# A two-MLP kernel after clustered attention: the reciprocal's correction on VectorE alone, weight splits moved between engines

## What is computed

```python
def _moe_ref(x, w_in, w_out, a, b):          # 1536 tokens, d_model 512, d_ff 2048
    h = x @ w_in
    P = a[0] + a[1]*h + a[2]*h*h + a[3]*h*h*h
    Q = 1.0 + abs(b[0])*abs(h) + abs(b[1])*h*h
    g = P / (Q + 1e-06)
    return g @ w_out

def _moe2_ref(x, w_gate, w_val, w_out):      # d_ff 1536
    g = x @ w_gate
    return (g / (1 + exp(-g)) * (x @ w_val)) @ w_out
```

## Time and profile before

| | us |
|---|---|
| median of three runs | 919.03 |
| the three runs | 916.78, 919.03, 922.4 |
| profiled execution, span of its instructions | 917.6 |
| TensorE matmul busy | 838.3 (91%) |
| VectorE busy | 575.2 (63%) |
| ScalarE busy | 475.2 (52%) |
| GpSimd busy | 417.9 (46%) |

### The profile page before, as it was taken

How to read it: one execution, slowest core, us unless ns; L and a number is a source line. 1 busy time by engine, 2 the same in 40 slices (tenths; PEclk the granted TensorE clock), 3 DMA queues, 4 the chain that set the end, 5 groups by cost and what they waited for, 6 DMA issues and landing times.

```text
span 917.6 us, 12016 instructions
## 1 busy us (share of the span) xinstructions
PE 838.3 (91%) x4210; PEld 710.1 (77%) x4210; DVE 575.2 (63%) x885; ACT 475.2 (52%) x898; POOL 417.9 (46%) x404
## 2 busy tenths in 40 slices
PE   5799889898999898888999899789999999999998
PEld 4698778888988676666888687667888888888886
DVE  2799888899999678877777778874322222122222
ACT  3588678777888576667666776753100100010001
POOL 3477787877758876656566666660000000000000
PEclk9999999999999999999999999999999999999999
DMA  3544323232332150000000023223000100010001
GB/s 95 150 112 106 90 69 91 67 100 68 93 82 61 61 169 1 1 0 1 1 1 0 1 70 94 79 69 103 1 1 1 46 0 1 1 46 1 0 1 46
DMA packets 44011, 45.38 MB, mean 49 GB/s; under 512 B 5040, under 2 KB 34736, under 8 KB 43952
## 3 DMA queue, kind: packets, MB, share of 16 engines
q1 hardware_dynamic: 43952, 44.62, 17.3%
HBM read 27.30 MB, written 3.15 MB: 33 GB/s over the span
## 4 chain that ended last, share of the span: by engine, by line
PE 47%; DVE 22%; POOL 12%; ACT 11%; issue 6%; POOLq 0%; DMA 0%; DVEq 0%; SPq 0%; ACTq 0%
PE ps L765 7%; PE ps L766 7%; PE ps L767 7%; POOL mag L373 6%; DVE den L619 4%; DVE neg_max L699 4%; PE ps L879 4%; PE ps L839 4%; PE ps L840 4%; PE ps L841 4%; DVE probT_lo L719 3%; POOL den L368 2%; ACT inv L480 2%; ACT inv L482 2%; DVE num L623 2%
## 5 line engine op out<-in xcount | busy, mean ns | idle before, releaser
L765 PE MATMUL ps<-x_hi,w_hi 128*128 128x512 f32 x480 | 187.1, 390 | 0.0
L766 PE MATMUL ps<-x_lo,w_hi 128*128 128x512 f32 x480 | 186.8, 389 | 0.0
L767 PE MATMUL ps<-x_hi,w_lo 128*128 128x512 f32 x480 | 186.7, 389 | 0.0
L666 DVE TENSOR_TENSOR act<-act,ps 128x512 f32<-128x512 f32 x36 | 24.8, 688 | 208.1 <-PE ps L767 206.1
L496 ACT ACTIVATE act<-ps 128x512 f32<-128x512 f32 x36 | 21.6, 599 | 243.0 <-PE ps L767 243.0
L373 POOL TENSOR_TENSOR mag<-mag,inv 128x512 f32<-128x512 f32 x48 | 81.4, 1695 | 79.6 <-ACT inv L482 79.6
L765 PE MATMUL ps<-g_hi,w_hi 128*128 128x512 f32 x192 | 79.0, 412 | 33.7 <-DVE g_lo L647 25.9
L395 POOL TENSOR_SCALAR prob<-prob,row_inv 128x768 f32<-128x768 f32 x96 | 85.7, 908 | 50.2 <-DVE row_inv L711 50.0
L719 DVE TENSOR_TENSOR probT_lo<-ps,probT_hi 128x384 fp32r<-128x384 f32 x192 | 97.4, 548 | 12.4 <-ACT probT_hi L528 12.0
L879 PE MATMUL ps<-ident,prob 128*128 128x128 f32 x576 | 82.9, 280 | 24.2 <-DVE probT_lo L719 22.4
L765 PEld LDWEIGHTS ps<-x_hi,w_hi 128*128 128x128 f32 x480 | 90.4, 188 | 18.8
(11 more groups left out here) (99 smaller groups left out, 1680.3 us busy)
## 6 DMA issues: line engine op xcount, KB each, us to landing
w_raw<-in_moe_w_out SPq DMA_DIRECT2D x28, 256.0 KB, 4.4
k_hihi<-qkT SPq DMA_DIRECT2D x32, 192.0 KB, 3.0
qk_low<-qkT SPq DMA_DIRECT2D x32, 192.0 KB, 3.7
w_raw<-in_moe_w_in SPq DMA_DIRECT2D x16, 256.0 KB, 3.9
qk_raw<-in_q SPq DMA_DIRECT2D x16, 192.0 KB, 2.7
qk_raw<-in_k SPq DMA_DIRECT2D x16, 192.0 KB, 2.6
v_raw<-in_v SPq DMA_DIRECT2D x16, 192.0 KB, 3.2
w_raw<-in_moe_w_gate SPq DMA_DIRECT2D x12, 256.0 KB, 3.0
```

The source lines that it names most:

```text
L765: mm(dst, hi, m_hi, start=start, stop=False)
L766: mm(dst, hi, m_lo, start=False, stop=False)
L767: return mm(dst, lo, m_hi, start=False, stop=stop)
```

## The change

The two corrections of the reciprocal are arranged anew. GpSimd keeps only den·mag. VectorE makes the product (den + 1 + 1e-6)·inv in one operation (`s_resid`), then inv = (that - 2)·inv, then g as before. ScalarE computes the magnitude and the linear part before num, and num gets a third buffer, with new waits for the shorter-lived buffers. The splits of ten first-MLP and twelve second-MLP weights leave ScalarE: the high part is a VectorE copy at the end of its step, and the low part is a subtraction by GpSimd behind its den·mag of that step. The core of the diff:

```diff
-    num = [place(f"num{i}", [P, TB]) for i in range(2)]
+    num = [place(f"num{i}", [P, TB]) for i in range(3)]
...
 # GpSimd, mlp1(n)
-                pool.wait_ge(s_lin, n + 1)
-                did(g.tensor_tensor(den[i][:, :], den[i][:, :], mag[i][:, :], ALU.mult), s_quad)
-                pool.wait_ge(s_quad, n + 1)
-                did(g.tensor_scalar(mag[i][:, :], den[i][:, :], DEN0, 1.0, ALU.add, ALU.mult), s_den1)
-                pool.wait_ge(s_den1, n + 1)
-                pool.wait_ge(s_inv0, n + 1)
-                did(g.tensor_tensor(mag[i][:, :], mag[i][:, :], inv[i][:, :], ALU.mult), s_newt)
+                if n < N1:
+                    pool.wait_ge(s_lin, n + 1)
+                    did(g.tensor_tensor(den[i][:, :], den[i][:, :], mag[i][:, :], ALU.mult), s_quad)
+                for u, when in w1_split_at.items():
+                    if when == n:
+                        pool.wait_ge(s_w1hi, u - POOL_UNITS + 1)
+                        did(g.tensor_tensor(w1_lo[u][:, :], w1_raw[u][:, :], w1_hi[u][:, :].bitcast(F32),
+                                            ALU.subtract), s_w1lo)
+                for j, when in w2_split_at.items():
+                    if when == n:
+                        pool.wait_ge(s_w2hi, j + 1)
+                        did(g.tensor_tensor(w2_lo[j][:, :], w2_raw[j][:, :], w2_hi[j][:, :].bitcast(F32),
+                                            ALU.subtract), s_w2lo)
...
 # ScalarE, mlps(n)
                     if n >= 2:
-                        sc.wait_ge(s_glo, n - 1)
+                        sc.wait_ge(s_quad, n - 1)
                     hid = ps[:, HID + n % 4, :]
-                    s.activation(num[i][:, :], hid, ACT.Identity, scale=a_neg[:, 3:4],
-                                 bias=a_neg[:, 2:3]).then_inc(s_num, 1)
                     s.activation(mag[i][:, :], hid, ACT.Abs).then_inc(s_mag, 1)
                     sc.wait_ge(s_mag, n + 1)
+                    if n >= 2:
+                        sc.wait_ge(s_inv1, n - 1)
                     s.activation(den[i][:, :], mag[i][:, :], ACT.Identity, scale=b_abs[:, 1:2],
                                  bias=b_abs[:, 0:1]).then_inc(s_lin, 1)
+                    if n >= 3:
+                        sc.wait_ge(s_glo, n - 2)
+                    s.activation(num[n % 3][:, :], hid, ACT.Identity, scale=a_neg[:, 3:4],
+                                 bias=a_neg[:, 2:3]).then_inc(s_num, 1)
...
-                for u, when in w1_split_at.items():
-                    if when == n:
-                        sc.wait_ge(s_w1_in[u], 32)
-                        s.activation(w1_hi[u][:, :], w1_raw[u][:, :], ACT.Copy).then_inc(s_w1hi, 1)
...
                     sc.wait_ge(s_quad, n + 1)
+                    if n >= 2:
+                        sc.wait_ge(s_g, n - 1)
                     s.activation(inv[i][:, :], den[i][:, :], ACT.Ln, bias=den0).then_inc(s_log, 1)
...
 # VectorE, mlps(n)
-                    ve.wait_ge(s_newt, n)
-                    v_.scalar_tensor_tensor(out=den[i1][:, :], in0=mag[i1][:, :], scalar=-2.0,
+                    i1, k1 = (n - 1) % 2, (n - 1) % 3
+
+                    ve.wait_ge(s_inv0, n)
+                    v_.scalar_tensor_tensor(out=den[i1][:, :], in0=den[i1][:, :], scalar=DEN0,
+                                            in1=inv[i1][:, :], op0=ALU.add, op1=ALU.mult
+                                            ).then_inc(s_resid, 1)
+                    ve.wait_ge(s_resid, n)
+                    v_.scalar_tensor_tensor(out=inv[i1][:, :], in0=den[i1][:, :], scalar=-2.0,
                                             in1=inv[i1][:, :], op0=ALU.add, op1=ALU.mult
                                             ).then_inc(s_inv1, 1)
...
                 for u, when in w1_split_at.items():
                     if when == n:
-                        ve.wait_ge(s_w1hi, u - POOL_UNITS + 1)
-                        v_.tensor_tensor(w1_lo[u][:, :], w1_raw[u][:, :], w1_hi[u][:, :].bitcast(F32),
-                                         ALU.subtract).then_inc(s_w1lo, 1)
+                        ve.wait_ge(s_w1_in[u], 32)
+                        v_.tensor_copy(w1_hi[u][:, :], w1_raw[u][:, :]).then_inc(s_w1hi, 1)
```

More of the change, by code:

```diff
@@ L177, in build_program @@
         "s_w1p_hi", "s_w1p", "s_w1hi", "s_w1lo", "s_w2hi", "s_w2lo"))
-    s_hid, s_num, s_mag, s_lin, s_num1, s_num2, s_quad, s_den1, s_log, s_inv0, s_newt = (
+    s_hid, s_num, s_mag, s_lin, s_num1, s_num2, s_quad, s_log, s_inv0, s_resid = (
         sem(x) for x in ("s_hid", "s_num", "s_mag", "s_lin", "s_num1", "s_num2", "s_quad",
-                         "s_den1", "s_log", "s_inv0", "s_newt"))
+                         "s_log", "s_inv0", "s_resid"))
     s_inv1, s_g, s_ghi, s_glo, s_y, s_yhi, s_ylo = (sem(x) for x in (
@@ L428, in _ @@
                     mlp1(TAIL[step])
-            for n in range(len(TAIL), N1):
+            for n in range(len(TAIL), N1 + N2 + 2):
                 mlp1(n)
@@ L474, in mlps @@
                         sc.wait_ge(s_y, n - 3)
-                    s.activation(g_hi[(n - 1) % 3][:, :], num[(n - 1) % 2][:, :], ACT.Copy
+                    s.activation(g_hi[(n - 1) % 3][:, :], num[(n - 1) % 3][:, :], ACT.Copy
                                  ).then_inc(s_ghi, 1)
@@ L615, in mlps @@
                 if 1 <= n <= N1:
-                    i1 = (n - 1) % 2
-                    ve.wait_ge(s_newt, n)
-                    v_.scalar_tensor_tensor(out=den[i1][:, :], in0=mag[i1][:, :], scalar=-2.0,
+                    i1, k1 = (n - 1) % 2, (n - 1) % 3
[5 more added lines that the diff above has]
+                    v_.scalar_tensor_tensor(out=inv[i1][:, :], in0=den[i1][:, :], scalar=-2.0,
                                             in1=inv[i1][:, :], op0=ALU.add, op1=ALU.mult
@@ L622, in mlps @@
                     ve.wait_ge(s_inv1, n)
-                    v_.scalar_tensor_tensor(out=num[i1][:, :], in0=num[i1][:, :], scalar=a_neg[:, 0:1],
-                                            in1=den[i1][:, :], op0=ALU.add, op1=ALU.mult
+                    v_.scalar_tensor_tensor(out=num[k1][:, :], in0=num[k1][:, :], scalar=a_neg[:, 0:1],
+                                            in1=inv[i1][:, :], op0=ALU.add, op1=ALU.mult
                                             ).then_inc(s_g, 1)
@@ L637, in mlps @@
                     ve.wait_ge(s_mag, n + 1)
-                    v_.tensor_tensor(num[i][:, :], num[i][:, :], hid, ALU.mult).then_inc(s_num1, 1)
+                    k = n % 3
+                    v_.tensor_tensor(num[k][:, :], num[k][:, :], hid, ALU.mult).then_inc(s_num1, 1)
                     ve.wait_ge(s_num1, n + 1)
-                    v_.scalar_tensor_tensor(out=num[i][:, :], in0=num[i][:, :], scalar=a_neg[:, 1:2],
+                    v_.scalar_tensor_tensor(out=num[k][:, :], in0=num[k][:, :], scalar=a_neg[:, 1:2],
                                             in1=hid, op0=ALU.add, op1=ALU.mult).then_inc(s_num2, 1)
@@ L646, in mlps @@
                     i3 = (n - 1) % 3
-                    v_.tensor_tensor(g_lo[i3][:, :], num[i1][:, :], g_hi[i3][:, :].bitcast(F32),
+                    v_.tensor_tensor(g_lo[i3][:, :], num[k1][:, :], g_hi[i3][:, :].bitcast(F32),
                                      ALU.subtract).then_inc(s_glo, 1)
@@ L678, in mlps @@
                     if when == n:
-                        ve.wait_ge(s_w2hi, j + 1)
-                        v_.tensor_tensor(w2_lo[j][:, :], w2_raw[j][:, :], w2_hi[j][:, :].bitcast(F32),
-                                         ALU.subtract).then_inc(s_w2lo, 1)
+                        ve.wait_ge(s_w2_in[j], 48)
+                        v_.tensor_copy(w2_hi[j][:, :], w2_raw[j][:, :]).then_inc(s_w2hi, 1)
             for step in STEPS:
```

## The result

The changed kernel takes 927.01 us (median of 6 runs, 925.17 to 928.62) against 920.53 us for the kernel before in the same comparison; the ratio is 1.0075, with a 95% interval of 1.0051 to 1.0098: 6.5 us slower. The forecast was 926.5 us. The profiled execution's span is 925.2 us, against 917.6.

What follows compares the result with a forecast made beforehand. A loop through g on VectorE, ScalarE and GpSimd was taken to hold TensorE back in the first MLP. Terms of 6.0 - 10.4 + 11.9 = +7.5 us gave a profiled 925.1 us, so 926.5 us forecast, range 919 to 934.

Steps and rivals of the forecast that it cites:

- First-MLP splits: Steps 3 to 12: a turn from g to g takes 7.80 instead of 7.13 us; nine turns, +6.0 us.
- The start: First longer turn, after g(2): costs nothing, since g(2) is done about 0.65 us earlier than now.
- The tail of attention: Attention's end: one VectorE operation more and two of GpSimd fewer per step, under half a microsecond either way.
- Middle: Steps 13 to 36: turns of 5.2 us, 129.4 us with two x_lo against 139.75 before, -10.4 us.
- rival C: Middle: product asked for after g, turn some 5.0 us until TensorE's 5.44 binds; 922 us, about no change; chance 0.18.
- Second-MLP splits: Steps 37 to 47, eight with splits: turns of 9.15 us, 87.9 us against 76.0 before, +11.9 us.
- Rival A: Split steps: GpSimd's low parts don't hold VectorE, turns 5.65 and 5.95 us; 882 us, faster; chance 0.12.
- Rival B: Middle: operations keep colliding, turn stays at 5.82 us; +10.4 on the forecast, 937 us; chance 0.15.

## Why the prediction was right

The mechanism of all three terms holds, and their sizes to about 1 us each. *First-MLP splits*: the turn is 7.68 instead of 7.80 us, the term +5.4 instead of +6.0. The low part asks while the residual runs, gets in before the correction, and the product behind it goes before g: order and holds are as written, and the weights put back (6.21) and the operation doubled (8.86) move the turn both ways. The start was off: g(2) was to be done 0.65 us earlier and so pay for the first longer turn. It ends at 332.88 instead of 332.96, 0.08 us earlier. The tail of attention, put at under half a microsecond, gives g(0) 1.4 us later against attention's last x_raw (3.62 us from its start at 316.69, and 2.20 from 316.41 before), and step 2 takes this back (5.83 instead of 7.61 us). So ten turns count, not nine: 10 x 0.55 less 0.1 is the +5.4. Nine of them alone would have been +5.0, so this error and that of the turn's length partly cancel. *Middle*: 5.20 us a turn, as forecast, with the product (508.98 to 510.28) cutting in before g (509.05 to 510.81); term -9.8 instead of -10.4. A part was off here: at the second block's end the loop waited for TensorE (VectorE idle 1.86 us until ScalarE's x_hi),

```profile
521.67 2.48 DVE L639 TENSOR_TENSOR x_lo<-ps,x_hi 128x512 fp32r<-128x512 f32 x4 [1.86 <-ACT x_hi L471]
```

and the step took 9.40 us where I had added 2.3 to 5.2; two shorter turns ahead of it (4.2 and 4.8) gave most of that back. Those two are the forecast's rival C setting in: the loop has caught up with TensorE, ScalarE's magnitude starts later, and the product is asked for when g has already begun, so g is no longer held:

```profile
514.25 0.75 DVE L631 SCALAR_TENSOR_TENSOR num<-num,par,inv 128x512 f32<-128x512 f32 x1
...
514.41 1.75 POOL L369 TENSOR_TENSOR den<-den,mag 128x512 f32<-128x512 f32 x1 [4.14 <-ACT den L460]
```

*Second-MLP splits*: 9.05 instead of 9.15, term +11.0 instead of +11.9; the estimates for the operations that the trace lacked, 0.69, 0.96 and 3.42 us, were within 0.08 us. The copy's 0.69 was a choice between 0.43 and 1.22 us, and that it came out exact is luck.

On TensorE's side I had forecast waits of about 2.2 us for g_lo in the first kind of split; there are 1.21 us for g_lo and 0.43 us for the low part of the weight. The wait for the low part I hadn't foreseen. It costs nothing, since TensorE waits for g_lo behind it all the same. The 3.5 us of the second kind came as 3.3 us, but only three times.

That these sum to +7.5 against +7.6 in span is partly luck: the three terms came out 0.9 us less in all, and the lower clock behind the last wait, which had no term of its own, gave 1.0 us back.

What the prediction lacked is the judgement of one part. Magnitude first stood in it only as the moment at which the product is asked for, and I took the 5.2 us turn that follows as the gain of the removed operations. That reordering by itself costs 9 to 14 us. The gain in the middle comes with the rearranged reciprocal (two GpSimd operations fewer, one of VectorE's more), and is 3.6 us larger without the reordering.

Rival A (no hold) is settled against: a doubled operation holds twice, a shorter one less. Rival B didn't happen: the middle turns are 5.20 us, not 5.8. The forecast's rival C happened in part. It set in at step 32 of the changed kernel, too late to matter; the kernels with num first, whose middle turns are 4.82 us, run into TensorE's 5.44, and so does the changed kernel with the second MLP's weights put back, from step 28.

## What to carry to other kernels

Where VectorE reads two inputs from SBUF, or copies there, and GpSimd works from SBUF too, count their operations as one queue: work moved from a busy VectorE to an idle GpSimd still takes VectorE's time (here 2.3 us for what VectorE did in 1.2), and falls wherever the other engine's dependent operations leave a crack. Ask of each GpSimd operation what VectorE does at that moment, and place it beside operations that read PSUM; being released earlier can be a loss, as the magnitude first shows. Take a change of several parts apart before keeping it: here one part was worth 40 us and two others cost 48.

## What the runs showed of the hardware

- A GpSimd operation with one SBUF input (weight times a constant, 0.93 us without its wait) holds a two-input VectorE operation until it is done: 1.42 instead of 0.69 us. The Trainium skill (SBUF — State Buffer, "SBUF: two separate sides") has the pair locked for the whole instruction whichever engine starts; the trace agrees for GpSimd operations of 0.9 to 3.4 us, and VectorE's held operation ends 0.53 to 0.56 us after each.
- VectorE's copy of 1024 float32 columns from SBUF takes 0.69 us, little more than half of the 1.22 us of a two-input operation, and it holds GpSimd: the product that takes 1.26 us alone took 1.65 us beside it, and ended 1.15 us after it.
- The two VectorE operations that read the hidden slice from PSUM (0.67 to 0.69 and 0.75 us) kept their length beside every GpSimd operation, in all twelve traces.
- Where an engine's next operation and the other engine's waiting one both hung on the same end, the one on the same engine got in first, in the kernel with the weights moved alone: GpSimd's low part started 0.07 us before VectorE's correction, released by the same product.
